# Attention's opening rebuilt: loads by pairs of heads, sums of four formed by TensorE, masks made first, local values loaded as 96 rows and the rest

## The reference, cut to what matters

```python
# q, k, v: (batch 4, heads 8, seq 576, head_dim 64), fp32
q_d = q.reshape(B, H, 144, 4, D).mean(axis=3)      # k_d, v_d the same
out_d = softmax(scale * q_d @ k_d.T) @ v_d         # pooled attention, 144 x 144
out_up = np.repeat(out_d, 4, axis=2)
mask = abs(pos[:, None] - pos[None, :]) < 4        # local attention, a band of 7
out_local = softmax(where(mask, scale * q @ k.T, -1e9)) @ v
x = out_up + out_local                             # -> (2304, 512)
# then: 8 experts, each token in one by a greedy choice with a cap; then a wide layer
```

## Time and profile before

| | |
|---|---|
| time before, median of 3 runs | 909.21 us (908.54 to 911.75) |
| the profiled execution's own time | 908.71 us |
| its span | 906.9 us |
| PE / PEld busy | 94% / 83% |
| DVE / ACT / POOL busy | 69% / 36% / 16% |
| attention, up to its last store of rows | 0 to about 196 us |

### The profile page before, as it was taken

The page is one execution under the profiler, slowest core; times in us unless marked ns, Lnnn a source line. Parts: engine busy times, 40 slices in busy tenths (PEclk is TensorE's granted clock), DMA queues, the critical chain, the costliest instruction groups (busy, mean ns, idle before and its releaser), DMA issues.

```text
span 906.9 us, 19254 instructions
## 1 busy us (share of the span) xinstructions
PE 848.2 (94%) x7220; PEld 754.7 (83%) x7220; DVE 624.8 (69%) x1706; ACT 327.9 (36%) x1041; POOL 144.9 (16%) x186
## 2 busy tenths in 40 slices
PE   7999999952899999999999999999999999999996
PEld 6677878651898899899889888998898899899995
DVE  5495867458889867876786567668767866875432
ACT  2767786722443242142134112421331242143111
POOL 5655645300000100110020001100200110010001
PEclk9999999965799999999999999999999999999999
DMA  7777651042653320430132021303400430340000
GB/s 165 156 166 180 159 133 55 10 120 88 192 176 89 111 94 1 123 120 2 53 122 71 1 80 55 114 1 95 118 30 1 139 104 2 93 149 3 1 1 35
DMA packets 122676, 77.27 MB, mean 85 GB/s; under 512 B 64280, under 2 KB 105240, under 8 KB 122584
## 3 DMA queue, kind: packets, MB, share of 16 engines
q1 hardware_dynamic: 119416, 65.83, 26.3%
q0 software_dynamic: 3168, 10.23, 3.6%
HBM read 66.59 MB, written 9.44 MB: 84 GB/s over the span
## 4 chain that ended last, share of the span: by engine, by line
PE 73%; DVE 15%; ACT 5%; issue 4%; DMA 1%; SPq 1%; POOL 0%; DVEq 0%; ACTq 0%; POOLq 0%
PE banks L969 19%; PE banks L971 18%; PE banks L970 18%; ACT prob L554 4%; DVE onehot L1298 2%; DVE neg L1341 2%; PE banks L386 2%; PE banks L990 2%; PE banks L974 2%; PE banks L975 1%; PE banks L290 1%; PE banks L398 1%; PE banks L354 1%; PE banks L415 1%; PE banks L277 1%
## 5 line engine op out<-in xcount | busy, mean ns | idle before, releaser
L1523 ACT CAST hid<-act 128x256 fp32r<-128x256 f32 (+1 forms) x128 | 55.5, 433 | 338.4 <-DVE act L1343 334.1
L969 PE MATMUL banks<-xy,win 128*128 128x256 f32 (+1 forms) x448 | 136.1, 304 | 2.1 <-DVE act L1343 2.1
L971 PE MATMUL banks<-xy,win 128*128 128x256 f32 (+1 forms) x448 | 132.6, 296 | 0.0
L970 PE MATMUL banks<-xy,win 128*128 128x256 f32 (+1 forms) x448 | 132.5, 296 | 0.0
L1341 DVE TENSOR_SCALAR neg<-banks,alph 128x256 f32<-128x256 f32 (+1 forms) x128 | 66.1, 517 | 92.9 <-PE banks L971 80.5
L969 PE MATMUL banks<-wout,hid 128*128 128x512 f32 x288 | 117.0, 406 | 1.2 <-DVE hid L1349 1.0
L970 PE MATMUL banks<-wout,hid 128*128 128x512 f32 x288 | 113.5, 394 | 0.0
L971 PE MATMUL banks<-wout,hid 128*128 128x512 f32 x288 | 112.9, 392 | 0.0
L1558 POOL DMA_INDIRECT rows<-x_rows,id_new x24 | 23.4, 976 | 505.4 <-DVE id_new L1306 500.5
L554 ACT ACTIVATE prob<-banks,nbias 96x102 f32<-96x102 f32 (+1 forms) x256 | 85.6, 349 | 16.9 <-DVE nbias L474 9.5
L969 PEld LDWEIGHTS banks<-xy,win 128*128 128x128 f32 x448 | 85.1, 190 | 6.1 <-DVE act L1343 3.1
(11 more groups left out here) (207 smaller groups left out, 1862.8 us busy)
## 6 DMA issues: line engine op xcount, KB each, us to landing
raw<-in_moe_w SPq DMA_DIRECT2D x128, 256.0 KB, 3.8
qn<-in_q SPq DMA_DIRECT2D x48, 96.0 KB, 2.5
kn<-in_k SPq DMA_DIRECT2D x48, 96.0 KB, 2.5
vn<-in_v SPq DMA_DIRECT2D x8, 576.0 KB
x_rows<-xs SPq DMA_DIRECT2D x24, 192.0 KB, 2.6
raw<-in_moe_w_in SPq DMA_DIRECT2D x16, 256.0 KB, 3.9
raw<-in_moe_w_out SPq DMA_DIRECT2D x16, 256.0 KB, 3.6
vw<-in_v SPq DMA_DIRECT2D x16, 204.0 KB
```

What stands on the lines that cost most here:

```text
L969: nc.tensor.matmul(out_ap, a_hi, b_hi, start=start, stop=False)
L970: nc.tensor.matmul(out_ap, a_lo, b_hi, start=False, stop=False)
L971: return nc.tensor.matmul(out_ap, a_hi, b_lo, start=False, stop=stop)
L1523: nc.scalar.copy(hid[:, (FC + j) % 3, 0, 0:CHUNK[k]], act[:, j % 2, 0:CHUNK[k]]).then_inc(h_hi, 1)
```

## The change

Six edits, all in attention's first turns, and one in every batch:

1. Loads of batch 0: a DMA takes one pair of heads (48 KB) where it took two pairs (96 KB), and so there are 48 for 24. v for the first half of the heads goes out ahead of the last pair. Each pair has semaphores of its own, one for q and one for k.
2. Sums by fours of batch 0: beside the three transposes, a unit with c = 0 now has six products (96 x 128 weights, the queries or keys as loaded, times a 96 x 24 matrix of ones and zeros, `fours`), which give the 144 sums in the same bank; DVE copies them out (`dve_pool_first`), and the `pool` steps of batch 0 are gone, with their eight reductions.
3. The plan: one pair of heads a turn in turns -3 to 0, where it was two, one and one; in turn 0 the flips of item 0 stand before the last pair's units; up to turn 0 DVE takes the maxima before it inverts; the pooled v of the second half moves to turn 0.
4. Fillers of L277 stand ahead of the scores of items 0 to 5.
5. POOL makes the masks before the constants for the routing, and the ones before both.
6. Local values, all batches: each of the six DMAs becomes two, of 96 rows and of the 6 (or 3) rows that are left.

```diff
-            first = {-LAG: (0, 1), 1 - LAG: (2,), 2 - LAG: (3,)}.get(t, ())
-            for hp in first:
-                qk(0, hp, all_four)
+            if t == 0:
+                self.steps += [("flip", t, 0), ("flip", t, 1)]
+            if t + LAG < HP:
+                qk(0, t + LAG, all_four)
...
+            if t <= 0:
+                self.steps.append(("max", t + LAG, 0))
             if 0 <= t + LAG - 1 < NU:
                 self.steps.append(("normalize", t + LAG - 1, 0))
...
+    def load_first_qk(e, hp):
+        heads = slice(2 * hp, 2 * hp + 2)
+        for t, (dst, src) in enumerate(((qn, q), (kn, k))):
+            for r in range(R):
+                e.dma_start(dst[:, r, heads], src[0, heads, r * T:(r + 1) * T].rearrange("h p d -> p h d")
+                            ).then_inc(qk_first[t][hp], 16)
...
-            e.dma_start(vw[lo:hi, b % 2, j, :].rearrange("p (h d) -> p h d", h=H),
-                        vt[b, s0:s0 + hi - lo]).then_inc(vw_in[b % 2], 16)
+            for a, z in ((lo, lo + T), (lo + T, hi)):
+                e.dma_start(vw[a:z, b % 2, j, :].rearrange("p (h d) -> p h d", h=H),
+                            vt[b, j * T - PAD + a:j * T - PAD + z]).then_inc(vw_in[b % 2], 16)
...
-        load_qk(e, 0, 0)
-        load_qk(e, 0, 1)
+        for hp in range(HP - 1):
+            load_first_qk(e, hp)
         load_v(e, 0, 0)
+        load_first_qk(e, HP - 1)
         load_v(e, 0, 1)
...
+        if b == 0 and c == 0:
+            if (t, hp) == (0, 0):
+                e.wait_ge(fours_made, 1)
+            for r in range(R):
+                at = S // 2 + r * (T // FACTOR)
+                last = nc.tensor.matmul(bank[:, at:at + T // FACTOR], (qn, kn)[t][:, r, 2 * hp:2 * hp + 2, :].rearrange("p h d -> p (h d)"),
+                                        fours[:], start=True, stop=True)
...
-            e.wait_ge(consts["fixed_made"], consts["ones_at"])
-        if 2 <= u <= LAG + 2:
+            e.wait_ge(consts["ones_made"], 1)
+        if u <= LAG + 2:
             pe_dense(psum[:, 512 * 7:512 * 8], 3)
...
+    def dve_pool_first(e, unit):
+        t, hp, _ = unit
+        e.wait_ge(flipped, PLAN.flipped("qk", 0, unit))
+        sums = pF[PLAN.place["qk", 0, unit] % RING][:, S // 2:S // 2 + SD]
+        if t == 0:
+            dve_copy(qdT[:, 0, hp, :], sums, SCALE)
+        else:
+            dve_copy(kdT[:, 0, hp, :], sums, None).then_inc(pooled_qk, 1)
```

More of the change, by code:

```diff
@@ L36, in qk @@
             self.steps += [("qk", b, (t, hp, c)) for t, c in units]
-            if units[-1] == (1, 1):
+            if b > 0 and units[-1] == (1, 1):
                 self.steps.append(("pool", b, hp))
@@ L51, in __init__ @@
                 self.steps.append(("exp", t + LAG - 1, 0))
-            if 0 <= t < NU:
+            if 0 < t < NU:
                 self.steps += [("flip", t, 0), ("flip", t, 1)]
+            if t <= 0:
+                self.steps.append(("max", t + LAG, 0))
             if 0 <= t + LAG - 1 < NU:
                 self.steps.append(("normalize", t + LAG - 1, 0))
-            if t in (1 - LAG, 2 - LAG):
-                self.steps += [("pool_v", 0, 3 * (t + LAG - 1) + stage) for stage in range(3)]
-            if 0 <= t + LAG < NU:
+            if t in (1 - LAG, 3 - LAG):
+                self.steps += [("pool_v", 0, 3 * (t + LAG - 1) // 2 + stage) for stage in range(3)]
+            if 0 < t and t + LAG < NU:
                 self.steps.append(("max", t + LAG, 0))
@@ L154, in attention @@
     mask = sb("mask", [T, 3, 4, W], BF16)
+    fours = sb("fours", [T, T // FACTOR], F32)
     ident, ident16 = consts["ident"], consts["ident16"]
@@ L165, in attention @@
     qk_in = [sem("qk_in0"), sem("qk_in1")]
+    qk_first = [[sem(f"{t}_first{hp}") for hp in range(HP)] for t in "qk"]
+    fours_made = sem("fours_made")
     vn_in, wg_in = [sem("vn_in0"), sem("vn_in1")], sem("wg_in")
@@ L214, in load_windows @@
             lo, hi = (PAD if j == 0 else 0), (W - PAD if j == NT - 1 else W)
-            s0 = j * T - PAD + lo
-            e.dma_start(vw[lo:hi, b % 2, j, :].rearrange("p (h d) -> p h d", h=H),
-                        vt[b, s0:s0 + hi - lo]).then_inc(vw_in[b % 2], 16)
+            for a, z in ((lo, lo + T), (lo + T, hi)):
+                e.dma_start(vw[a:z, b % 2, j, :].rearrange("p (h d) -> p h d", h=H),
+                            vt[b, j * T - PAD + a:j * T - PAD + z]).then_inc(vw_in[b % 2], 16)
     def store_x(e, b, j):
@@ L282, in pe_qk @@
         t, hp, c = unit
-        if (t, c) == (0, 0) and hp % (HP // 2) == 0:
-            e.wait_ge(qk_in[hp // (HP // 2)], 16 * 2 * R * (b + 1))
+        if b == 0 and c == 0:
+            e.wait_ge(qk_first[t][hp], 16 * R)
+        elif (t, c) == (0, 0) and hp % (HP // 2) == 0:
+            e.wait_ge(qk_in[hp // (HP // 2)], 16 * 2 * R * b)
         pe_bank_free(e, "qk", b, unit)
@@ L321, in pe_scores @@
             if u == HP:
+                for c in range(2):
+                    wait_emptied(e, "qk", 0, (1, HP - 1, c))
                 e.wait_ge(masks_made, 1)
@@ L378, in pe_apply @@
             if x == 0:
-                e.wait_ge(vw_in[b % 2], 16 * NT * (b // 2 + 1))
+                e.wait_ge(vw_in[b % 2], 16 * 2 * NT * (b // 2 + 1))
             e.wait_ge(summed, b * NT + x)
@@ L505, in vector @@
     def vector(e):
+        e.wait_ge(consts["made"], 2)
+        nc.vector.tensor_reduce(fours[:], ident[0:T, 0:T].rearrange("p (m r) -> p m r", r=FACTOR), AX.X, ALU.add
+                                ).then_inc(fours_made, 1)
         nc.vector.memset(kT[:, :, :, 0:PAD], 0.0).then_inc(pads_made, 1)
@@ L511, in vector @@
             if kind == "qk" and x[2] == 0:
+                if u == 0:
+                    dve_pool_first(e, x)
                 empty_qk(e, dve_copy, u, x).then_inc(emptied_dve, 1)
@@ L616, in pool_norm, with gpsimd @@
             nc.gpsimd.tensor_tensor(p, p, inv.unsqueeze(2).to_broadcast([rows, heads, width]), ALU.mult).then_inc(normed, 1)
-    def gpsimd(e):
+    def gpsimd(e, make_fixed):
         band = consts["pool_steps"]
@@ L635, in gpsimd @@
         nc.gpsimd.memset(consts["spare"][:], 0.0).then_inc(masks_made, 1)
+        make_fixed(e)
         for kind, u, x in STEPS:
@@ L678, in make_route_consts @@
     g.iota(f["row_at"][:, 2, :], pattern=[[0, E]], base=1, channel_multiplier=1, allow_small_or_imprecise_dtypes=True).then_inc(made, 1)
-    n, tiles, at, cut_at = 8, NT * T // TILE // B, 0, 0
-    for t in ("ones", "segment", "before"):
+    n, tiles, at, cut_at = 7, NT * T // TILE // B, 0, 0
+    for t in ("segment", "before"):
         g.memset(f[t][:], 1.0).then_inc(made, 1)
@@ L1652, in attention_then_experts @@
     NT = B * S // T
-    N_CONSTS = 12 + len(set(DIGIT_BITS)) + 2 * B
+    N_CONSTS = 11 + len(set(DIGIT_BITS)) + 2 * B
     with ExitStack() as whole, ExitStack() as first:
@@ L1673, in attention_then_experts @@
         psum = [banks[:, 512 * i:512 * (i + 1)] for i in range(8)]
-        ident_made, fixed_made = sem("ident_made"), sem("fixed_made")
+        ident_made, ones_made, fixed_made = sem("ident_made"), sem("ones_made"), sem("fixed_made")
         consts = dict(ident=ident, ident16=ident16, spare=spare, made=ident_made, n_made=4,
-                      ones=fixed["ones"], fixed_made=fixed_made, ones_at=8,
+                      ones=fixed["ones"], ones_made=ones_made,
                       pool_steps=sem("mask_steps"))
@@ L1725, in _ @@
                 n += 1
-            make_route_consts(nc, e, fixed, T, NT, E, J, TILE, SLOTS, B, fixed_made)
-            attn["gpsimd"](e)
+            nc.gpsimd.memset(fixed["ones"][:], 1.0).then_inc(ones_made, 1)
+            attn["gpsimd"](e, lambda e: make_route_consts(nc, e, fixed, T, NT, E, J, TILE, SLOTS, B, fixed_made))
             moe["gpsimd"](e)
```

## The result

The changed kernel takes 915.99 us, median of 14 runs (911.59 to 924.23), against 909.02 of the kernel before in 14 runs beside them (905.95 to 915.09). The ratio is 1.0083, with a 95% interval of 1.0063 to 1.0103: slower, by 7.0 us, where the forecast of 912.8 lay 3.6 over the median of before that was shown. By the bands that the prediction names (slower from 913.8 on) this is slower, to which it gave 0.30. Its profiled execution took 921.11 us, and 908.71 was that of before.

A forecast was written before the change was run, and what follows sets the result against it. PE was taken to bound the opening, moving the end of item 3's exponentials from 31.8 to 35.9 us; the other parts counted 0, so 908.7 + 4.1 = 912.8 us, range 907.5 to 916.

The forecast's parts named there:

- the bands that the prediction names: Whole kernel: below 904.7 us faster (0.06), above 913.8 us slower (0.30), between them same (0.64).
- The path that it forecast: Opening: PE works without gaps from 7.9 us to pair 4's last unit at 31.8, then 4.1 us to item 3's inversion.
- the sum: Whole kernel: 908.7 us plus 4.1 gives 912.8 us.
- the stated range: Whole kernel: 907.5 to 916 us, leaving out the combined fast case and the clock's tail.
- The gate: End of item 3's exponentials, where DVE inverts their sums: 35.9 us against 31.8; the kernel moves by as much.
- each product instruction 0.112: Batch 0's units on PE: 12 product instructions at 0.112 us, 1.34 us a unit, 10.7 us in all.
- The rival of cheap products: Opening: weight loads cost the transpose's 0.083 us, so loads of keys bound; 910 to 911.4 us, chance 0.22.
- The start of PE: Opening: PE starts where the 18 fillers end, 7.9 us, where before it waited until 9.03 for keys.
- Loads by pairs: Batch 0's loads on SP: 0.52 us an issue, last keys usable at 28.4 us, hidden by 1.1 us.
- Local values: Local loads on SP, all batches: about 7 us against 14.98; worth 0 on the path, at most 4.4 us.
- Masks and order: POOL makes masks first and works in another order: 0, nothing above 0.2 either way.
- The rival's paragraph: Opening, now PE's: two stretches of low granted clock, 1.7 us each, give 916.2 us; chance 0.15.

The follow-up runs named there:

- e1_wide: Changed kernel with each product of the sums moving 96 columns in place of 24, the further 72 being zeros: 913.13 us, ratio 1.0039.
- e7_wide_no_fillers: Changed kernel with products moving 96 columns and without the filler ahead of each of batch 0's units: 912.54 us, ratio 1.0056.
- e3_local_loads_only: Kernel before with only the local values' loads split as in the change, in all batches: 909.36 us, ratio 1.0005.
- e6_order_only: Changed kernel with batch 0's sums made by DVE, no products, and the loads of before: 911.62 us, ratio 1.0018.
- e4_no_unit_fillers: Changed kernel without the filler product ahead of each of batch 0's sixteen transposing units: 915.34 us, ratio 1.0068.
- e8_products_only: Kernel before with only batch 0's sums by 24-column products and DVE's copies, no reductions; loads, order and fillers of before: 927.38 us, ratio 1.02.
- v1_merged: Changed kernel with transposes and sums merged into products moving 120 columns, no unit fillers, loads of before, sums copied by DVE and ACT: 906.11 us, ratio 0.9963.
- e2_no_products: Changed kernel with batch 0's sums made by DVE again and no products, all else of the change kept: 914.34 us, ratio 1.0068.

## Where the prediction held, and the step that failed

The path that it forecast was right and can be seen by itself in e1_wide. What failed was the price of that path: the sum takes all of PE's work in the opening at full clock, and puts a fall of the clock at nothing because PE would be fuller. The runs show a fall in a full PE, worth 8.3 us in the profiled execution and 2.3 of the median's 7.0. The median, 915.99, still lies 0.01 us inside the stated range; that is luck, since the range was meant to leave the clock's tail out.

- **The gate, and that the shift goes through whole: right.** Own time less gate is 876.1 in after and 876.9 before, and 876 to 880 in all twelve kernels, the upper ones with falls of the clock behind the gate.
- **The opening is bound by PE, each product instruction 0.112: right.** In the chain of waits of after twelve last 1.28 us at full clock, 0.107 each (first row below), and 2.44 at half (second row). The Trainium skill, "TensorE: Matmul & The Clock Gate", section "LDWEIGHTS (loading the stationary operand)", would have a load last its columns divided by 1.2 ns, here 107 ns. The pace of the narrow products agrees (0.107 us from one to the next), though the records of these loads last 0.188 us or more each, and the transposes, which load 128 columns as well, follow at 0.083. With 96 columns moved twelve last 1.34 us in e1_wide, the forecast's 0.112 each. The rival of cheap products, 0.083 each, is refuted.

```profile
21.99 1.28 PE banks L314 x12
31.94 2.44 PE banks L314 x12
```

- **The start of PE, 7.9 us: off by 0.9 to 1.1.** With its filler ahead, the first unit's transposes would have begun at 8.15; they came at 9.05 in e1_wide and 9.29 in after. The 18 fillers at the start took longer there: the granted clock was full from 5.5 us in before's execution, from 7.6 in e1_wide's and from 8.1 in after's. Before has no unit to run ahead of 9.03, when its keys have come, so there a late clock would be hidden up to then. This is the 0.8 us by which e1_wide's gate misses 35.9.
- **Loads by pairs, 0.52 us an issue, hidden: right.** Six take 2.92 us on SP in after (0.49 each), the last keys' issues start at 22.84, and with or without them the gate is 36.7 and 36.9. That they are hidden by little was right as well: e7_wide_no_fillers uncovers them for 2.11 us. It was the queries of the last pair that came late there, though, not the keys that the sum watches.
- **Local values: worth 0, shown by e3_local_loads_only.** SP needs 8.67 us in after where I took 7. Masks and order were put at 0, and no run tests either alone. Order, added fillers and masks together cost 1.2 us when DVE does the sums (e6_order_only); in e1_wide, behind a full PE, nothing of that is seen, since the late start accounts for its 0.8 us.
- **The step that failed: the clock.** The rival's paragraph argued "Against: 1.00 from 10 to 15 us with PE at 3.71 of 5, and PE will be fuller". PE was fuller, 5.00 of 5, and the clock fell all the same, in after from 25.2 to 42.2. The argument had one kind of fall before it, the one that comes after idle time (before's PE is busy 2.78 of 4 us from 32 to 36, and its clock falls at 36.2), and took it for the only one. Half of after's stretch is 8.5 us; the gate is 44.98 - 36.69 = 8.3 us later than in e1_wide, where the clock stayed. I had given this 0.15, and sized it as two stretches of 1.7 us, 3.4 in all; it was two and a half times that. By the runs' mean clocks it isn't one case or the other either: against the four runs at 0.972 and more, the seven of the middle group take 3 to 6 us longer and the last three 9 to 12. The median, 915.99, lies in the middle group, 3.2 us above the forecast. These clocks are means of whole executions, and before's runs have them from 0.961 to 0.975 too; where the clock fell is known for the profiled executions only.
- **What the clock answered to.** Two pairs of kernels differ in the width of the products alone. With 96 columns moved the profiled execution kept its clock through the opening (e1_wide, e7_wide_no_fillers); with 24 it lost it (after at 25.2 us, e4_no_unit_fillers at 18.0), and so did e8_products_only at 15.5. PE was busy all the time from 9.3 us up to each of these three falls, so its busy share doesn't tell them from e1_wide. The runs say the same less sharply. The mean clock is 0.970 or more in 4 of 14 runs of after against 7 of 9 of e1_wide, and in none of 6 of e4_no_unit_fillers against 7 of 12 of e7_wide_no_fillers. Of before's runs it is 34 of 71, but it was 6 of 17 in one round and 21 of 34 in another, so these counts are a weak ruler; e8_products_only, with all six runs below any of before, is clear without them. So it is shown that the loss is more frequent and longer with the narrow products. It isn't shown why, and wide ones don't rule it out. Single falls of 3.4 to 10 us occur in other kernels too (39.5 to 42.9 in v1_merged, 44 to 54 in e6_order_only), and what sets them off stays open.

## What to carry to other kernels

A product with a wide weight and few columns costs its weight load, so it isn't cheap, and a PE full of such products can lose half its clock. Give them the wider moving operand, which cost 0.06 us in twelve instructions here and made the loss rarer, or merge them with a product that loads the same weight anyway. When work is moved to the engine that is to become the bound, price it at both clock levels. Find the one instruction through which the shift must pass: own time less that instant told in one profile what a median could only blur. And before a difference of two profiles is put down to the edit between them, compare the granted clock of both up to that instruction: 1.27 us of e2_no_products looked like late loads and was one stretch of half clock.

## What the runs showed of the hardware that was not expected

- With PE busy 5.00 of 5 us throughout, the granted clock still went to 0.5 for 17.1 us (after), 23.9 us (e4_no_unit_fillers) and 30.7 us (e8_products_only).
- The first rise of the clock varies from execution to execution with the same 18 fillers: 5.5, 7.6 and 8.1 us in before, e1_wide and after, with the first filler at 2.1 us in each.
- The issue of a load on SP lasts 0.49 us for half the bytes that took about 0.5 before: on this queue the price was per issue.
- A load of 48 KB issued after v's landed 4.90 us after its issue (e7_wide_no_fillers); the keys at the start of before, 96 KB, took 2.50.
- Twelve fp32 products on 128-column weights last 1.28 us with 24 columns moved (after) and 1.34 with 96 (e1_wide).
